# A gated scan and an ELU feed-forward layer: matmul operands stored in the order in which the passes read them

## What is computed

```python
def _attn_ref(x, f_logit, lower_bound):
    sig = 1.0 / (1.0 + np.exp(-f_logit))
    f = lower_bound[None, None, :] + (1.0 - lower_bound[None, None, :]) * sig
    i = 1.0 - f
    for t in range(S):
        h = f[:, t] * h + i[:, t] * x[:, t]
        y[:, t] = h

def _moe_ref(x, w_in, w_out):          # w_in 256 x 2048, w_out 2048 x 256
    h = x @ w_in
    g = np.where(h > 0.0, h, alpha * (np.exp(np.minimum(h, 0.0)) - 1.0))
    return (g @ w_out).astype(np.float32)
```

## Time and profile before

| | |
|---|---|
| median of 3 runs | 961.72 us |
| profiled execution | 962.05 us |
| its span | 960.2 us |
| TensorE matmuls, busy | 954.3 us, 4362 of them |
| TensorE weight loads, busy (beside the matmuls) | 815.4 us |
| ScalarE, busy | 790.1 us |
| VectorE, busy | 722.3 us |
| GpSimd, busy | 628.8 us |
| DMA | 42.02 MB, 44 GB/s on the mean |
| granted TensorE clock | 1.00 of full speed |

### The profile page before, as it was taken

One profiled execution on the slowest core, in us unless ns is written; L12 is line 12 of the kernel. 1 busy time (PEld: TensorE's weight loads), 2 busy tenths in 40 slices (PEclk: granted clock), 3 DMA queues, 4 the chain that ended last, 5 costly groups with the idle time before them and its releaser, 6 DMA issues.

```text
span 960.2 us, 15016 instructions
## 1 busy us (share of the span) xinstructions
PE 954.3 (99%) x4362; PEld 815.4 (85%) x4362; DVE 722.3 (75%) x916; ACT 790.1 (82%) x1424; POOL 628.8 (65%) x477
## 2 busy tenths in 40 slices
PE   9999999999999999999999999999999999999998
PEld 6999888888888888888888888888888888888887
DVE  6998876976886796697688679679768867966444
ACT  7989888878888888888888888888888788887775
POOL 2578796576667668557656755856775765676544
PEclk9999999999999999999999999999999999999999
DMA  7212012002101201100210210120021021001001
GB/s 273 68 33 95 0 34 66 34 1 78 55 1 55 77 1 44 55 33 1 75 55 0 66 66 0 45 66 20 23 65 44 0 76 55 0 0 46 1 1 45
DMA packets 23078, 42.02 MB, mean 44 GB/s; under 512 B 2560, under 2 KB 4096, under 8 KB 23040
## 3 DMA queue, kind: packets, MB, share of 16 engines
q1 hardware_dynamic: 22752, 41.10, 13.2%
q10 hardware_dynamic: 288, 0.46, 0.1%
HBM read 29.10 MB, written 12.45 MB: 43 GB/s over the span
## 4 chain that ended last, share of the span: by engine, by line
PE 96%; ACT 2%; DVE 1%; issue 1%; POOL 0%; ACTq 0%; POOLq 0%
PE acc L896 17%; PE acc L898 17%; PE acc L897 17%; PE h L868 14%; PE h L866 14%; PE h L867 14%; ACT e L472 1%; PE h L1010 1%; PE h L1002 1%; PE h L1004 1%; PE h L1003 1%; ACT e L466 1%; DVE x L628 0%; PE h L968 0%; ACT w_out_hi L505 0%
## 5 line engine op out<-in xcount | busy, mean ns | idle before, releaser
L336 POOL TENSOR_TENSOR g_lo<-e,g_hi 128x512 fp32r<-128x512 f32 (+1 forms) x384 | 516.4, 1355 | 325.5 <-ACT g_hi L480 324.0
L466 ACT ACTIVATE e<-h 128x512 f32<-128x512 f32 (+1 forms) x379 | 224.8, 593 | 124.6 <-PE h L868 90.3
L719 DVE SCALAR_TENSOR_TENSOR e<-e,h 128x512 f32<-128x512 f32 (+1 forms) x379 | 256.8, 678 | 70.2 <-ACT e L472 69.1
L896 PE MATMUL acc<-g_hi,w_out_hi 128*128 128x512 f32 (+1 forms) x768 | 291.1, 379 | 0.4 <-DVE w_out_lo L690 0.4
L898 PE MATMUL acc<-g_hi,w_out_lo 128*128 128x512 f32 (+1 forms) x768 | 291.0, 379 | 0.0
L897 PE MATMUL acc<-g_lo,w_out_hi 128*128 128x512 f32 (+1 forms) x768 | 290.9, 379 | 0.0
L472 ACT ACTIVATE e<-e 128x512 f32<-128x512 f32 (+1 forms) x384 | 241.3, 628 | 9.7 <-issue 1.2
L480 ACT CAST g_hi<-e 128x512 fp32r<-128x512 f32 (+1 forms) x384 | 232.1, 604 | 19.3 <-DVE e L719 19.3
L866 PE MATMUL h<-a_hi,w_in_hi 128*128 128x512 f32 x616 | 234.7, 381 | 0.0
L868 PE MATMUL h<-a_hi,w_in_lo 128*128 128x512 f32 x616 | 234.7, 381 | 0.0
L867 PE MATMUL h<-a_lo,w_in_hi 128*128 128x512 f32 x616 | 234.7, 381 | 0.0
(11 more groups left out here) (77 smaller groups left out, 556.0 us busy)
## 6 DMA issues: line engine op xcount, KB each, us to landing
opening<-forget_logit SPq DMA_DIRECT2D x44, 256.0 KB, 2.7
x<-value SPq DMA_DIRECT2D x44, 256.0 KB, 2.7
out<-out_sb SPq DMA_DIRECT2D x44, 256.0 KB, 2.0
w_in_raw<-w_in SPq DMA_DIRECT2D x8, 256.0 KB, 5.4
w_out_raw<-w_out SPq DMA_DIRECT2D x8, 256.0 KB, 6.5
out<-out_sb SPq DMA_DIRECT2D x4, 224.0 KB, 1.9
x<-value SPq DMA_DIRECT2D x3, 224.0 KB, 6.1
opening<-forget_logit SPq DMA_DIRECT2D x2, 224.0 KB, 6.3
```

The lines of the kernel that those rows point to most:

```text
L336: nc.gpsimd.tensor_tensor(g_lo[:, t % RING, 0:w], e[:, t % TILES, 0:w], g_hi[:, t % RING, 0:w].bitcast(F32), ALU.subtract).then_inc(g_lo_r ...
L466: nc.scalar.activation(e[:, i, 0:w], bank_of(j, t)[:, 0:w], ACT.Relu, scale=-1.0).then_inc(r_ready, 1)
L719: nc.vector.scalar_tensor_tensor(e[:, t % TILES, 0:w], e[:, t % TILES, 0:w], -1.0, bank_of(j, t)[:, 0:w], ALU.add, ALU.max).then_inc(g_rea ...
L896: nc.tensor.matmul(bank, hi, g_h, start=opens, stop=False)
```

## The change

In blocks 1 to 11 the rows `a_hi`, `a_lo`, `g_hi` and `g_lo` are stored in the order in which the passes take them: first the 128 columns of the first pass, then those of the second, and so on. For this, the instructions that write these rows (ScalarE's `split` and `round_g`, GpSimd's `rest_g` and `rest`, VectorE's `rest`) read their source, `e` or a piece of `y`, through the view `in_order`, and write their result straight on. The subtractions have two sources: the plain one is read through the view, the `hi` row straight on. The matmuls of `product` and `second` now read 512 contiguous columns, and write their bank through the view as before, so that the tokens lie in PSUM in the same places as before. Block 0 is unchanged, and so are the number and the sequence of the instructions, the waits and the DMAs.

```diff
+def row_order(columns, j):
+
+    if isinstance(j, int) and j == 0:
+        return columns
+    return columns
+
+def token_order(columns, j):
+
+    if isinstance(j, int) and j == 0:
+        return columns
+    return in_order(columns)
...
             def rest_g(j, t):
-                nc.gpsimd.tensor_tensor(g_lo[:, t % RING, 0:w], e[:, t % TILES, 0:w],
-                                        g_hi[:, t % RING, 0:w].bitcast(F32),
+                nc.gpsimd.tensor_tensor(row_order(g_lo[:, t % RING, 0:w], j),
+                                        token_order(e[:, t % TILES, 0:w], j),
+                                        row_order(g_hi[:, t % RING, 0:w].bitcast(F32), j),
                                         ALU.subtract).then_inc(g_lo_ready, 1)
...
             def rest(j, par, product):      # GpSimd, and the same on VectorE
-                nc.gpsimd.tensor_tensor(lo[:, 0:w], unsplit(j, product, w), hi[:, 0:w].bitcast(F32),
+                nc.gpsimd.tensor_tensor(row_order(lo[:, 0:w], j), token_order(unsplit(j, product, w), j),
+                                        row_order(hi[:, 0:w].bitcast(F32), j),
                                         ALU.subtract).then_inc(a_lo_ready[product], 1)
...
             def split(j, par, product):
-                nc.scalar.copy(a_parts(par, product)[0][:, 0:w], unsplit(j, product, w)).then_inc(a_hi_ready, 1)
+                nc.scalar.copy(row_order(a_parts(par, product)[0][:, 0:w], j),
+                               token_order(unsplit(j, product, w), j)).then_inc(a_hi_ready, 1)
...
             def round_g(j, t):
-                nc.scalar.copy(g_hi[:, t % RING, 0:w], e[:, t % TILES, 0:w]).then_inc(g_hi_ready, 1)
+                nc.scalar.copy(row_order(g_hi[:, t % RING, 0:w], j),
+                               token_order(e[:, t % TILES, 0:w], j)).then_inc(g_hi_ready, 1)
...
             def product(j, par, q, k, bank, start=False):
-                into = in_order(bank[:, 0:w])
-                a_h, a_l = in_order(a_h[:, 0:w]), in_order(a_l[:, 0:w])
+                into = token_order(bank[:, 0:w], j)
+                a_h, a_l = row_order(a_h[:, 0:w], j), row_order(a_l[:, 0:w], j)
...
             def second(j, t, half):
-                bank, g_h, g_l = in_order(bank), in_order(g_h), in_order(g_l)
+                if first:
+                    bank, g_h, g_l = in_order(bank), in_order(g_h), in_order(g_l)
+                else:
+                    bank, g_h, g_l = token_order(bank, j), row_order(g_h, j), row_order(g_l, j)
```

More of the change, by code:

```diff
@@ L655, in rest @@
                 hi, lo = a_parts(par, product)
-                nc.vector.tensor_tensor(lo[:, 0:w], unsplit(j, product, w), hi[:, 0:w].bitcast(F32),
+                nc.vector.tensor_tensor(row_order(lo[:, 0:w], j), token_order(unsplit(j, product, w), j),
+                                        row_order(hi[:, 0:w].bitcast(F32), j),
                                         ALU.subtract).then_inc(a_lo_ready[product], 1)
```

## The result

The changed kernel takes 988.39 us (988.32 to 988.92, 4 runs) against 961.82 us for the kernel before: ratio 1.0278, 95% interval 1.0265 to 1.0292. It is slower by 2.8%. Six executions, one of the kernel before here (1004.4 us), two of it beside later runs (1004.3 and 1004.5) and three of the ten of `read_passes` (1004.5 to 1005.1), are some 43 us longer than the others of the same kernel and are left out of the ratios; the paragraph on what stays open comes back to them.

The account below looks back on a forecast made before the run. TensorE was taken to bound the kernel, with 3960 products at 220 ns and no waits. All terms were taken as 0, so the span stayed 960.2 us and the forecast median was 961.7 us, range 944 to 990.

Parts of the forecast that it names:

- What bounds the kernel: Blocks 1 to 11: TensorE never waits for data; time is 3960 products times 220 ns between starts, 871.2 us.
- Terms 2 to 5: ScalarE casts, GpSimd and VectorE subtractions reading in passes, and the kernel's end: each taken as 0.
- Term 1: TensorE's 3960 products in blocks 1 to 11, now read straight: taken as 0, bounds -15.8 and +39.6 us.
- the 4 ns: Gap between warm-up bf16 products (216 ns) and the layer's (220); candidates: read passes, write passes, four-byte data.
- The slower rival: Straight reads in blocks 1 to 11 meet weight loads: 1 to 10 ns a product, 5 taken, 981.5 us; chance 0.31.
- The faster rival: Reading in passes carries the 4 ns per product, so straight reads give 945.9 us; chance 0.30.
- The bound above: Term 1's upper limit, from block 0 products at 203.8 against 193.6 ns: 10 ns more each, +39.6 us.

Follow-up runs that it names:

- read_passes: Against the kernel before, blocks 1 to 11 write rows through the view, read them in passes and write PSUM straight on: 961.95 us, ratio 0.9988.
- bench1: TensorE alone, no layer computed, 27 groups of 48 products in different read and write orders: straight reads 226.8 ns, 4 passes of runs of eight 230.9.
- straight_both: Against the changed kernel, blocks 1 to 11 also write PSUM straight on, with no view left on any engine: 988.64 us, ratio 1.0254 to the kernel before.
- bench5: TensorE alone, 25 groups of 48 products with weights' steps, weights' or rows' places and row lengths varied: straight reads 226.7 ns, up to 244.4 with every 8th weight column.
- weights_128: The kernel before with all weights 128 bytes further on in SBUF and every row read where it was: 1001.42 us, ratio 1.0414.
- bench6: TensorE alone, 16 groups, mostly 512 columns read in 4 passes of runs of eight, after different lead-ins: 220.0 or 230.7 ns for the same products.

## Why the prediction was wrong

**What bounds the kernel** was read rightly. There is no wait of TensorE before or after, and 3960 times the change of the distance is the change of the time.

**Terms 2 to 5** were right: the casts and subtractions didn't grow, and the end didn't move.

**Term 1 failed, at the step "I take 0".** The argument was that the 4 ns between the bf16 row and the layer's rows had three possible causes, of which two stay. `bench1` and `straight_both` show that one of them, the write passes, never had a part. The other two act in opposite directions: from bf16 to fp32r, both read straight, the distance goes from 216 to 226.7 ns, and the read passes take 6.7 of that back. The 4 ns were the difference of these two, and a cause that lowers the distance was not among the candidates. The term was +26.6 us where 0 was taken. `bench5` and `weights_128` show besides that the excess isn't a property of a pattern alone: it also hangs on what is loaded beside the read. The comparison with the warm-up couldn't show this, since bf16 has half the bytes and a shorter load, 97 ns beside 188. A straight fp32r read was no mixture of those rows but a third case, 226.7 ns.

**The slower rival was what happened.** It put straight reads that meet the weight loads at 1 to 10 ns a product and took 5, for 981.5 us; measured are 6.6 ns and 988.4 us, inside the range of 944 to 990. Its direction was right, but the row that spoke for it, block 0 at 50 to 52 us, showed something else (below), so that the size came near was luck. That weight loads matter to the distance is shown (`weights_128`, `bench5`). Its picture of how they meet, that a straight read sweeps over all of the memory's parts as a load does, is not shown: shorter loads should have helped, and straight reads beside loads of 32 columns took 231.7 ns against 226.7.

**The faster rival** had read passes carry a cost. It is the reverse: the passes of runs of eight are what brings the distance from 226.7 to 220.

**The bound above** was taken from block 0, where products after a wait start every 203.8 ns instead of 193.6. I read it as a lasting effect of the position of loads against products. The trace shows a stretch of settling: ten distances of 198 to 210 ns follow that wait, up to the next one. After a later wait of block 0 such a stretch goes over to 193 and 194 ns at its sixteenth product, and most lead-ins of `bench6` do so too. It had no bearing on 3960 products that are never waited for. A lasting second value exists for 448 columns too, 200.0 ns in one lead-in of `bench6` (L178), but block 0 didn't stay there.

**The rules named, and the traces.** The Trainium skill's "PSUM — Partial Sum Buffer", section Specifications (TRN2), says that a pattern that isn't contiguous slows matmuls significantly. Here writes in runs of eight slow nothing: 3090 products in 700 us with and without them, 3183 and 3184 with reads in passes. By the Trainium skill's "GPSIMD Engine Reference", section 7, a step of 4 bytes inside a run is not charged, and the 1354 ns, against 1357 before, agree. The rule that spoke most against my slower rival, and which I had not weighed, is in the Trainium skill's "TensorE: Matmul & The Clock Gate", section "Step-by-step: what each phase is for": two independent read ports, so that loading the next weights doesn't take read bandwidth from the running matmul. `weights_128`, 4.1% slower with the same reads and another address of the weights, disagrees for fp32r, and the measurement decides.

**Open.** What is shown is which side of the product costs the time, and how much. Why is not: why reading in four passes of runs of eight can run at 220.0, why straight reads settle at 226.7, what picks a rhythm, and why shorter loads make it worse. The executions of about 1004 us fit the second rhythm, 961.8 + 3960 x 0.0107 = 1004.2. Only the kernel before and `read_passes`, which both read in passes, had them, at a granted clock of 0.998 to 1.00 in the five for which it is on record; the two kernels that read straight had none, though in 8 executions only. None of the six was profiled, so this is argued. If it is so, the changed kernel is slower than the fast rhythm of the kernel before and faster than its slow one.

## What to carry to other kernels

Where TensorE is never waited for, read the distance between starts, not the busy share, and try the order and the addresses of what it reads before anything else: here they were worth 2.8% and 4.1% with not one instruction more or less. A rate in one part of a trace may depend on what ran before it, so a measurement of a pattern by itself needs the lead-in that it has in the kernel. And before a bound is worked out from rows that differ in three things, run the one that differs in one.

## What the runs showed of the hardware

- The order in which an fp32r product writes PSUM (straight, or 4 passes of runs of eight) made no difference (3090 products in 700 us both ways, and 3183 and 3184); for bf16 neither side's order did (216 ns).
- Straight fp32r reads follow every 226.7 ns (512 columns), in 4 passes of runs of eight every 220.0. The gap doesn't grow with the columns: at 256 it is 120.0 and 113.3, the same 6.7 ns, but at 448 202.7 and 193.3, at 384 173.3 and 171.7, and at 320 both have 146.7.
- The distance changes with the address of the weights: for straight reads from 226.7 to 233.4 ns at 64 bytes on, 232.4 at 128 and 226.7 at 256; in the layer, 4x8, from 220.0 to 229.4 at 128. A straight row 32 bytes on had 233.3.
- Products in 4x8 have two lasting rhythms, 220.0 and 230.7 ns. Thirty straight products at 160 us are enough to bring the layer from one to the other for the 840 us that are left.
- ScalarE, VectorE and GpSimd read runs of eight of 32 columns as fast as a contiguous row (609, 1304 and 1354 ns against 608, 1310 and 1357).
